# Attention kernel with two feed-forward layers: the first query loads go out on ScalarE's queue

## What is computed

```
k_p = k.reshape(B, H, 72, 8, 64).mean(axis=3);  v_p likewise
scores = q @ k_p^T / 8;  attn = softmax(scores);  x = attn @ v_p
h = x @ w_in;   g = 0 if h <= -1, h if h >= 1, else (h + 1)^2 / 4;   x = g @ w_out
h = x @ w2_in;  g = max(h, 0) + log(1 + exp(-|h|));                 out = g @ w2_out
```

## Time and profile before

| | |
|---|---|
| median of three runs | 850.37 us |
| the profiled execution | 849.2 us, of it 847.4 us span |
| PE busy | 840.4 us, 99% of the span |
| DVE, ACT, POOL busy | 539.7, 496.6, 311.9 us |
| granted PE clock | 1.00 |

### The profile page before, as it was taken

How to read it: one execution, slowest core, us unless ns; L and a number is a source line. 1 busy time by engine, 2 the same in 40 slices (tenths; PEclk the granted TensorE clock), 3 DMA queues, 4 the chain that set the end, 5 groups by cost and what they waited for, 6 DMA issues and landing times. The chain is left out here.

```text
span 847.4 us, 13193 instructions
## 1 busy us (share of the span) xinstructions
PE 840.4 (99%) x5234; PEld 819.7 (97%) x5234; DVE 539.7 (64%) x611; ACT 496.6 (59%) x701; POOL 311.9 (37%) x289
## 2 busy tenths in 40 slices
PE   8999999999999999999999999999999999999998
PEld 7779999899999999999999999999999999999998
DVE  4884765622234587768657676666678896768641
ACT  3886665643445444453435987887788753535442
POOL 6885866655455600000000575474455500000000
PEclk9999999999999999999999999999999999999999
DMA  9944757564546895454623354676464996555532
GB/s 196 221 121 149 242 172 250 170 213 160 204 161 218 269 396 223 166 207 163 232 103 105 111 200 164 210 226 210 167 208 157 337 397 225 205 181 192 207 111 75
DMA packets 97726, 167.84 MB, mean 198 GB/s; under 512 B 21633, under 2 KB 85633, under 8 KB 93057
## 3 DMA queue, kind: packets, MB, share of 16 engines
q1 hardware_dynamic: 85352, 157.85, 55.0%
q10 hardware_dynamic: 12312, 9.14, 3.8%
HBM read 96.21 MB, written 70.78 MB: 197 GB/s over the span
## 5 line engine op out<-in xcount | busy, mean ns | idle before, releaser
L1275 PE MATMUL ps<-xs,W 128*128 128x384 f32 x2304 | 406.7, 335 | 0.1
L1275 PEld LDWEIGHTS ps<-xs,W 128*128 128x128 f32 x2304 | 398.6, 188 | 4.3 <-issue 3.9
L1293 PE MATMUL ps<-xs,Tm 128*128 128x384 f32 x1968 | 344.0, 334 | 0.2 <-DVE xs L1015 0.2
L1293 PEld LDWEIGHTS ps<-xs,Tm 128*128 128x128 f32 x1968 | 340.7, 188 | 0.5 <-issue 0.5
L777 ACT ACTIVATE xs<-ops 128x768 fp32r<-128x768 f32 (+1 forms) x148 | 111.7, 826 | 159.9 <-PE ps L1293 159.9
L633 POOL TENSOR_TENSOR ops<-ops 128x384 f32<-128x384 f32 x48 | 60.9, 1270 | 330.9 <-DVE ops L1087 255.4
L1015 DVE TENSOR_TENSOR xs<-ops,xs 128x768 fp32r<-128x768 f32 (+1 forms) x148 | 130.2, 940 | 0.0
L1067 DVE SCALAR_TENSOR_TENSOR ops<-ps,t_a 128x768 f32<-128x768 f32 x48 | 45.9, 956 | 108.8 <-ACT t_a L801 108.6
L799 ACT ACTIVATE t_a<-ps 128x768 f32<-128x768 f32 x48 | 39.0, 812 | 95.4 <-PE ps L1275 95.3
L1100 DVE TENSOR_TENSOR X<-ps,X 128x768 f32<-128x768 f32 x41 | 38.7, 956 | 83.7 <-PE ps L1293 83.7
L1082 DVE SCALAR_TENSOR_TENSOR ps<-ps,t_b 128x768 f32<-128x768 f32 x48 | 46.4, 966 | 31.5 <-ACT t_b L824 31.5
(11 more groups left out here) (89 smaller groups left out, 623.6 us busy)
## 6 DMA issues: line engine op xcount, KB each, us to landing
gops<-ops SPq DMA_DIRECT2D x48, 1344.0 KB, 5.8
ops<-gops SPq DMA_DIRECT2D x36, 1536.0 KB, 6.7
X<-gops SPq DMA_DIRECT2D x22, 384.0 KB, 6.4
w_raw<-in_moe_w_in_dram SPq DMA_DIRECT2D x16, 512.0 KB, 4.6
t_raw<-in_moe_w_out_dram SPq DMA_DIRECT2D x6, 1024.0 KB, 10.0
out_dram<-y_out ACTq DMA_DIRECT2D x11, 384.0 KB, 2.6
k_raw<-in_k_dram SPq DMA_DIRECT2D x10, 288.0 KB
q_raw<-in_q_dram SPq DMA_DIRECT2D x20, 144.0 KB, 7.3
```

The costliest lines, as they stand in the source:

```text
L1275: last = mm(banks[:, tb, :], W[:, slot, part, c, f * P:(f + 1) * P], x[:, x_part, at:at + TB], start=c == 0 and s == 0, stop=c == KC - 1 a ...
L1293: last = mm(banks[:, d, :], Tm[:, t, part, j, d * P:(d + 1) * P], g[:, g_part, at * TB:(at + 1) * TB], start=at == 0 and s == 0, stop=at = ...
```

## The change

ScalarE issues the two DMAs of q for unit 0 as its first instructions, ahead of the table load. After the table load, and ahead of `copy_qk(0)`, it issues the six DMAs of q for units 1 to 3. SyncE no longer issues these eight; its list starts with k0, k1, k2, k3, v0, and goes on with k4, q4 as before. The buffers and the semaphores are the same. In `load_q`, which is now called for units 4 and up alone, the wait is written without the helper that leaves out waits for zero.

```diff
             def load_q(u):
-                wait(sp, qk_transposed, u - 3)
+                sp.wait_ge(qk_transposed, u - 3)
...
             for u in range(PAIRS):
                 load_k(u)
-                load_q(u)
             load_v(0)
...
         def _(act):
+
+            def first_q(u):
+                for h in range(2):
+                    act.dma_start(q_in(u)[:, :, h, :], q_src[u, h]).then_inc(q_loaded[u % PAIRS], 16)
+
+            first_q(0)
             act.preload_act_table_set("natural_log_exp_and_others")
...
+            for u in range(1, PAIRS):
+                first_q(u)
             copy_qk(0)
             for i in range(-1, FIRST + 2):
                 turn(i)
```

## The result

The changed kernel takes 859.37 us (median of 20 runs, 858.08 to 867.17) against 850.08 us for the kernel before (20 runs, 849.15 to 863.29): a ratio of 1.010, with a 95% interval of 1.008 to 1.012. The forecast was 851.1 us with a range up to 854.6; the time lies well outside it, on the slow side, by 9.3 us where 0.7 was forecast.

What follows compares the result with a forecast made beforehand. The prediction took PE to bound the kernel, with no gaps to catch up in. Its terms, 0 + 0.7 + 0 + 0 + 0 = +0.7 us on a median of 850.37, gave 851.1 us, range 849.7 to 854.6.

Steps and rivals of the forecast that it cites:

- What bounds the kernel: Whole kernel: PE sets the pace; earlier loads give back almost nothing, a delay of unit 0's chain moves everything behind it.
- Part 2: k0's load, sharing engines with q0: lands 1.1 us later, making PE 0.7 us late, range 0 to 1.1 us.
- Part 3: q0's load beside SyncE's loads: 600 pieces per us, landing at about 5.7 us, not late; cost 0.
- the other mode: q0's load, Part 3: engines serve in order of issue, k1, k2 and perhaps k3 first; q0 lands at 7.5 to 8.6.
- Part 4: ScalarE's issues before copy_qk(0): done at about 7.5 us, hidden by 0.4 us; a hold possible but not taken, cost 0.
- Rival 1: ScalarE held at its own queue while PE, DVE and POOL wait for its copy: +1.5 to +4.3 us, chance 0.22.
- Rival 3: Start of PE: rival 1's hold so long that the clock falls back, 5.8 us more, 856.2 us; chance 0.06.

Runs made afterwards that it cites:

- e7: Changed kernel with more padding matmuls on PE, 31 ahead of the first transposes and 8 behind them instead of 11 and 3: 855.01 us, ratio 1.006.
- e9: Changed kernel with q laid out head by head, moving in 1536-byte instead of 256-byte pieces, for timing alone: 850.02 us against 849.98, ratio 1.000.
- e11: Kernel before, all loads on SyncE's queue, with q in the same long pieces of 1536 bytes, for timing alone: 849.23 us against 849.98, ratio 0.998.
- e2: Kernel before with one wait added on PE ahead of the first transposes, for the second unit's summed keys; loads unchanged: 857.5 us against 850.03.
- e1: Changed kernel with 26 padding matmuls on PE instead of 11 ahead of the first transposes: 859.09 us, ratio 1.013.
- e4: Changed kernel with SyncE waiting behind k0 until q0 has landed, before issuing k1, k2, k3 and v0: 851.65 us against 850.03.
- e3: Kernel before with only q0 moved to ScalarE's queue, ahead of the table load: 855.87 us against 850.03, ratio 1.006.
- e6: Changed kernel with ScalarE's q1 to q3 issued behind copy_qk(0) instead of ahead of it: 860.38 us against 849.86, ratio 1.013.

## Why the prediction was wrong

**What bounds the kernel** was right: PE sets the pace, an earlier load gives nothing back, and a later start is hardly caught up. With the clock up, e7 is 5.2 us over the kernel before for first scores 5.8 us later, and e9 is 0.8 us over its counterpart e11 for 1.0 us.

**Part 2** expected k0 late by 1.1 us and PE by 0.7. k0 was late by 0.33 (4.40), within the slack of its k_pair. Even that need not be the second queue's doing: e2, whose loads are those of the kernel before, has 4.36. Wrong in size, and it carried the whole forecast.

**Part 3 is the step that failed.** It let q0 run at 600 pieces per us beside another queue, taken from the earlier trace rows. Measured: 244. The rate was read from one stretch of 1.5 us, with other traffic in SyncE's queue: 151 packets of 1.2 KB on average, which took 37% of the engines, where here the five loads of 2 KB pieces took 62%. SyncE's queue was not empty in that stretch either. A store issued before that stretch, at 96.46 us, landed only after it, at 105.9 (the kernel before; the last columns are KB and us to landing):

```profile
gops<-ops SPq DMA_DIRECT2D x1, 1344.0 KB, 9.4
```

Why ScalarE's queue got 77% of the engines there, and 30% in the changed kernel, no run shows. And the prediction held the opposite sign in its hands: in the earlier trace rows ScalarE's queue moved nothing for 2 us beside SyncE's loads. It used this for k0, as a lower bound, and not for q0. It had the other mode, service behind what is issued earlier, as a bound that put q0 at 8.6 at the latest; it landed at 10.6.

**Part 4** named the hold and its row rightly and then took none, by the same rate. At 244 per us 2700 pieces need 11 us, and the last issue would end at about 13.4; it ended at 12.55. Its upper bound for the copy, 11.5 us, was 1.2 us short (12.72).

**Rival 1** had the mechanism of ScalarE's hold, with a chance of 0.22, and was wrong on what it costs: where PE is late by itself the hold adds 1.1 us (e1), and in the profiled execution nothing, since ScalarE's last issue ended at 12.55 and PE's transposes at 12.68.

**Rival 3** had the fall of the clock and gave it 0.06. Its price, 1.5 us from 22 padding matmuls, was that of one short stretch. (It follows from the busy times, 4.46 us for 22 at the start against 1.3 for 10 later; the two means, which overlap, would give 3.6.) The clock stayed down far longer, and the median cost is about 4.4 us. Its condition, that ScalarE come free only after 14 us for a loss over 1%, was wrong too: ScalarE was free at 12.55 and the loss was 9.3 us, over 1%, which had a chance of 0.03. An idle time of 3.4 us alone lost 7.5 us (e2).

**The Trainium skill** (DMA: Bandwidth & Descriptors, "Issuing engines are not separate DMA queues") had DMAs from different engines run on the same 16 DMA engines and interleave. That agrees, and the total of 219 GB/s agrees with almost no gain from a second queue; but "no gain" is not "no loss". The same page's rule that the engines go round the queues packet by packet ("Queues, rings and completion order") means by a packet a group of several descriptors. The packets counted in the profile are single pieces, so the rule can't be checked in these rows. They show the outcome alone: nearly one for one in e9 (343 to 374), and about three short pieces for one long in the changed kernel (1954 to 615).

## What to carry to other kernels

A load put in a second queue gets an earlier issue but loses its place in line: beside a backed-up queue of long pieces, one of short pieces gets a small part of the bytes. Before moving the load that everything waits for, count what the other queue will now issue ahead of time, and keep the order with a wait (e4, 1.6 us over the kernel before) or with one queue.
Don't take the rate of a shared stretch from one row: look at several, and at what kind of traffic stands in the other queue.
Price a gap on PE near the start by its length and by the clock that may fall behind it.

## What the runs showed of the hardware that I had not expected

- The clock stayed at half for some 33 us in the profiled execution of the changed kernel with PE busy throughout, and for some 13 us in e3; what ended it in each the runs don't tell. The mean granted clock of the changed kernel's executions is 0.98 in the longest (867.17 us) and 0.988 to 0.994 in all others but one, of 859.95 us, which has 1.0. So the mean does not tell of every execution how it ran; two of e3's four have 1.0 as well, with 854.07 and 856.88 us.
- It fell behind two short gaps of 0.77 and 0.63 us (e3), while in e4's profiled execution it stayed up behind 0.63 and 1.76 us, and in e9's behind 0.37 and 0.63. What tells them apart is open.
- In the changed kernel 1176 pieces had moved on ScalarE's queue by 6 us, about as many as q0 has, but q0's second half landed at 10.6. So some of them were probably q1's, which passed before the last of q0's. Without followers (e6) only 996 had moved by then, and yet q0 came a microsecond earlier, which agrees.
